# Query tiles' numerators one slot later, and first in TensorE's slot: a linear attention stage ahead of two expert layers

## The reference

```python
def phi(x):
    proj = np.einsum('bhsd,df->bhsf', x, w_phi)              # 64 -> 128 features
    proj = proj - np.max(np.abs(proj), axis=-1, keepdims=True)
    return np.concatenate([np.exp(proj), np.exp(-proj)], axis=-1)
q_p, k_p = (phi(q), phi(k))
kv = np.einsum('bhsf,bhsd->bhfd', k_p, v)
z = np.sum(k_p, axis=2)
num = np.einsum('bhsf,bhfd->bhsd', q_p, kv)
den = np.einsum('bhsf,bhf->bhs', q_p, z)[..., None] + 1e-06
return (num / den).astype(np.float32)
```

## Time and profile before

| | us |
|---|---|
| median of three runs | 910.85 (910.55 to 911.68) |
| the profiled execution, its own time | 910.34 |
| its span in the trace | 908.7 |
| TensorE busy, share of the span | 886.8, 98% |
| VectorE busy | 432.3, 48% |
| ScalarE busy | 293.9, 32% |
| GpSimd busy | 123.4, 14% |

### The profile page before, as it was taken

The page is one execution under the profiler, slowest core; times in us unless marked ns, Lnnn a source line. Parts: engine busy times, 40 slices in busy tenths (PEclk is TensorE's granted clock), DMA queues, the critical chain, the costliest instruction groups (busy, mean ns, idle before and its releaser), DMA issues.

```text
span 908.7 us, 15622 instructions
## 1 busy us (share of the span) xinstructions
PE 886.8 (98%) x5888; PEld 811.7 (89%) x5889; DVE 432.3 (48%) x875; ACT 293.9 (32%) x479; POOL 123.4 (14%) x145
## 2 busy tenths in 40 slices
PE   8999999999999999999999999999999999999996
PEld 6795968779999999999988999999999999999996
DVE  5678687898767644333457422222222222222222
ACT  4545454572155532223353321121112112112111
POOL 1010302122344112222300010010001001001001
PEclk9999999999999999999999999999999999999999
DMA  9513713112457432346743630030020002000000
GB/s 296 178 54 124 271 52 104 53 48 59 157 177 196 79 58 71 26 78 122 159 157 114 181 112 1 1 105 1 0 70 35 0 2 102 0 0 35 1 1 35
DMA packets 37181, 75.31 MB, mean 83 GB/s; under 512 B 8176, under 2 KB 24688, under 8 KB 35472
## 3 DMA queue, kind: packets, MB, share of 16 engines
q1 hardware_dynamic: 32832, 56.07, 23.2%
q0 software_dynamic: 3488, 17.85, 5.3%
q10 hardware_dynamic: 816, 0.79, 0.3%
HBM read 51.06 MB, written 23.64 MB: 82 GB/s over the span
## 4 chain that ended last, share of the span: by engine, by line
PE 89%; DVE 5%; issue 2%; ACT 2%; DMA 1%; POOL 0%; POOLq 0%; DVEq 0%; SPq 0%; ACTq 0%
PE ps L1023 10%; PE ps L1025 10%; PE ps L1024 10%; PE ps L822 6%; PE ps L1038 5%; PE ps L1039 5%; PE ps L1037 5%; PE ps L925 4%; PE ps L938 3%; PE ps L926 3%; PE ps L927 3%; PE ps L940 3%; PE ps L939 3%; PE ps L769 3%; PE ps L729 2%
## 5 line engine op out<-in xcount | busy, mean ns | idle before, releaser
L1023 PE MATMUL ps<-xnH,blkH 128*128 128x384 f32 x576 | 193.7, 336 | 3.0 <-DVE blkL L1690 1.9
L1025 PE MATMUL ps<-xnH,blkL 128*128 128x384 f32 x576 | 193.4, 336 | 0.0
L1024 PE MATMUL ps<-xnL,blkH 128*128 128x384 f32 x576 | 193.2, 335 | 0.0
L1697 DVE TENSOR_TENSOR sg<-sg,ps 128x384 f32<-128x384 f32 x72 | 39.8, 553 | 245.5 <-ACT sg L1256 241.6
L1256 ACT ACTIVATE sg<-ps 128x384 f32<-128x384 f32 x72 | 35.4, 491 | 252.1 <-PE ps L1025 252.1
L1023 PEld LDWEIGHTS ps<-xnH,blkH 128*128 128x128 f32 x576 | 108.2, 188 | 7.5 <-issue 4.3
L1024 PEld LDWEIGHTS ps<-xnL,blkH 128*128 128x128 f32 x576 | 108.2, 188 | 2.6
L1025 PEld LDWEIGHTS ps<-xnH,blkL 128*128 128x128 f32 x576 | 108.1, 188 | 0.0
L1038 PE MATMUL ps<-blkL,hH 128*128 128x512 f32 x216 | 84.8, 393 | 0.0
L1039 PE MATMUL ps<-blkH,hL 128*128 128x512 f32 x216 | 84.8, 392 | 0.0
L1037 PE MATMUL ps<-blkH,hH 128*128 128x512 f32 x216 | 84.5, 391 | 0.0
(11 more groups left out here) (219 smaller groups left out, 1593.6 us busy)
## 6 DMA issues: line engine op xcount, KB each, us to landing
stage<-in_ffn_w SPq DMA_DIRECT2D x12, 768.0 KB, 4.3
xin<-xs_dram SPq DMA_DIRECT2D x9, 578.2 KB, 9.9
xs_dram<-zrow SPq DMA_DIRECT2D x8, 578.2 KB, 8.6
qT<-in_q SPq DMA_DIRECT2D x4, 1152.0 KB, 5.5
xnH_dram<-xoH SPq DMA_DIRECT2D x8, 576.0 KB, 3.5
xnL_dram<-xoL SPq DMA_DIRECT2D x8, 576.0 KB, 6.1
xnH<-xnH_dram SPq DMA_DIRECT2D x6, 768.0 KB, 5.4
xnL<-xnL_dram SPq DMA_DIRECT2D x6, 768.0 KB, 6.3
```

Source lines behind the costliest of these rows:

```text
L1023: e.matmul(o, hi, xnH[par][:, c, :], start=(c == 0), stop=False)
L1024: e.matmul(o, hi, xnL[par][:, c, :], start=False, stop=False)
L1025: last = e.matmul(o, lo, xnH[par][:, c, :], start=False, stop=(c == KC - 1))
```

## The change

- `num_of`: the packed tile's numerators go to bank 2, one of the transposes' banks, and no longer to bank 6.
- TensorE: the numerators of a tile come three slots after its own (`g3`) and not two, as first half, projections, second half, ahead of the key sums and transposes. The packed tile's numerators (slot 2 of the next batch) stand between the two halves' projections with nothing between their own halves, and the second half's projections come ahead of the key sums there. In all other slots the second half's projections come last. Slot 7 has no numerators any more.
- VectorE: normalises the tile of four slots ago.
- The second wait in `key_sums` is gone; the first transposes of a batch wait for the previous batch's last normalisation in its place.
- The splits of the last batch move from its slots 1, 2, 5, 6, 7, 8, 9 to 2, 4, 5, 7, 8, 8, 9.
- The hand-over: `first_transposes` uses its banks in another order, waits for one tile of exponentials less, and for the last tile only ahead of bank 2. The numerators of slot 8's tile now come behind the first transposes, in `slot(B, 1)`, and the packed tile's behind the wait for `dve_XT`, in `slot(B, 2)`.

```diff
@@ num_of
-            first = KVB if at[1] % NJ % 2 == 1 else ZB
+            first = 2 if packed(at) else KVB if at[1] % NJ % 2 == 1 else ZB
@@
-        split_slots_dve = [(B - 1, sl) for sl in (1, 2, 5, 6, 7, 8, 9)] + [(B, 0)]
+        split_slots_dve = [(B - 1, sl) for sl in (2, 4, 5, 7, 8, 8, 9)] + [(B, 0)]
-        XT_FIRST = (2, 3, 1, 0)
+        XT_FIRST = (3, 1, 0, 2)
@@ key_sums
-                if j == 0 and not first:
-                    e.wait_ge(s["dve_N"], at[0] * NJ)
-                    settle(e, "carry_pe")
@@ numerators
-                    elif at[1] > NJ + 1:
+                    elif at[1] > NJ + 1 and not packed(at):
@@ TensorE's slot
-                g1, g2 = (before_slot(b, sl, n) for n in (1, 2))
+                g1, g2, g3 = (before_slot(b, sl, n) for n in (1, 2, 3))
-                turned = sl == NJ + 2 and has_slot(b)
-                if turned:
+                short = is_q(g3) and packed(g3)
+                if sl == NJ + 2 and has_slot(b):
                     turn(b)
+                if is_q(g3) and not short:
+                    numerators(g3, 0)
                 if has_slot(b):
                     projections(b, sl, 0)
+                if short:
+                    numerators(g3, 0)
+                if is_q(g3):
+                    numerators(g3, 1)
+                if short and has_slot(b):
+                    projections(b, sl, 1)
                 if is_k(g2):
                     key_sums(g2)
...
                     elif not (isinstance(g1[0], int) and g1[0] == 0):
                         e.wait_ge(s["act_Q"], g1[0] * NJ)
+                        e.wait_ge(s["dve_N"], g1[0] * NJ)
+                        settle(e, "carry_pe")
...
-                if is_q(g2) and not turned:
-                    numerators(g2, 0)
-                if has_slot(b):
+                if has_slot(b) and not short:
                     projections(b, sl, 1)
-                if turned:
-                    numerators(g2, 0)
-                if is_q(g2):
-                    numerators(g2, 1)
@@ first_transposes
                 for c in range(KC):
+                    if c == KC - 1:
+                        e.wait_ge(s["act_Q"], B * NJ)
                     x_transpose(c, XT_FIRST[c])
@@ hand-over, TensorE
-                e.wait_ge(s["act_Q"], B * NJ)
+                e.wait_ge(s["act_Q"], B * NJ - 1)
                 first_transposes()
             slot(B, 1)
             with e.If(early > 0):
                 e.wait_ge(s["dve_XT"], KC)
+            slot(B, 2)
+            with e.If(early > 0):
                 once(0, 0)
                 hidden(0, 0, 0)
...
-            for sl in range(2, TAIL_SLOTS):
+            for sl in range(3, TAIL_SLOTS):
@@ VectorE's slot
-                g3 = before_slot(b, sl, 3)
+                g4 = before_slot(b, sl, 4)
                 if sl == NJ + 2 and has_slot(b):
                     turned_evac(b)
-                if is_q(g3):
-                    normalise(g3)
+                if is_q(g4):
+                    normalise(g4)
...
-                    n = split_slots_dve.index((b, sl))
-                    split_low(n, 0, n + 1)
+                    for n, at in enumerate(split_slots_dve):
+                        if at == (b, sl):
+                            split_low(n, 0, n + 1)
```

## The result

| | before | after |
|---|---|---|
| median of 8 runs each, same chips | 910.58 us | 914.56 us |
| lowest to highest | 909.9 to 911.68 | 913.13 to 916.32 |
| ratio, 95% interval | | 1.0043 [1.0033, 1.0054] |
| profiled execution, time (span) | 910.34 (908.7) | 915.47 (913.9) |
| mean granted clock of TensorE, profiled | 0.999 | 0.988 |

The forecast was 908.9 us, the range 906.4 to 911.2. What came is rival (c), to which the prediction gave 0.06: 913.8 forecast for it, 914.56 measured.

The account below looks back on a forecast made before the run. TensorE, busy 98% at full clock, was taken as the bound. Gains of 4.7 + 1.2 us, less 0.9 + 0.6 at and after the borders and 2.5 at the hand-over, made 1.9 us less: 908.9 us, range 906.4 to 911.2.

Parts of the forecast that it names:

- rival (c): Idle time ahead of the first transposes drops TensorE's clock to 1.2 GHz; numerators behind take twice as long, 913.8 us; chance 0.06.
- The borders: At three borders between batches, TensorE's waits lose 4.6 to 4.7 us; the change leaves 0.9 us of that.
- the second waits: TensorE's slot 3 waits for a low part at the borders, 0.29 us at the one shown; they would go.
- The new order on TensorE: Fewer entries into fast runs and packed numerators in one run save 0.4 us a border, 1.2 us in all.
- The last batch: Moved splits delay VectorE: slot 5's projections 0.25 us late, `turn` 0.35 us late, 0.6 us more in all.
- The hand-over's wait: Ahead of the experts' first transposes TensorE idles 3.1 us, from 217.08 us until they start at 220.2 us.
- my chain of 12.65 us: VectorE's steps without pause from 203.42 us until slot 6's rows are normalised at 216.1 us.
- Nothing overlaps: At the hand-over, GpSimd's copy (0.6), VectorE's last split (1.14) and the gating (2.03) run one after another, until 220.0 us.
- the term of the hand-over: At the hand-over to the experts, `hidden` starts 1.85 us later, plus a 0.65 us wait: 2.5 us lost.
- The 0.65 us for `early_low(0)`: After two chunks of hidden rows, TensorE waits 0.65 us for VectorE's late `early_low(0)`.
- (a): The hand-over hides: transposes start near 218.5 us, loss there under 1 us, time 907.1 us; chance 0.22.
- (b): Waits move and don't go: half the border gain, 2.2 us, comes back as waits, time 911.1 us; chance 0.22.

Follow-up runs that it names:

- experiment 1: The changed kernel with 29 extra fast matmuls, results unused, ahead of the first transposes; 908.03 us against 909.31 for the kernel before.
- experiment 4: The changed kernel with the numerators of slot 8's tile back ahead of the first transposes; 905.65 us against 909.31 for the kernel before.
- experiment 3: The changed kernel with the last batch's splits back in slots 1, 2, 5, 6, 7, 8, 9; 910.9 us, 1.0008 of the kernel before.
- experiment 6: The kernel of experiment 4 with the packed numerators back in bank 6 and the key sums' second wait restored; 916.45 us, 1.0084 of the kernel before.
- experiment 2: The changed kernel with GpSimd gating the experts' first rows ahead of copying slot 6's tile; 910.94 us, 1.0013 of the kernel before.
- experiment 5: The kernel before, with GpSimd's gating put behind the copies of three tiles and not two; 911.78 us against 909.35.
- experiment 7: The changed kernel with 15 extra fast matmuls, results unused, ahead of the first transposes; 912.51 us, 1.0035 of the kernel before.
- experiment 9: The changed kernel with 16 extra fast matmuls, results unused, right behind the first transposes; 912.96 us, 1.0035 of the kernel before.

## Why the prediction was wrong, point by point

**The borders: right.** "Left over at the borders: 3 x 0.3 = 0.9 us" measured 0.19, 0.22 and none, 0.41 in all; the second waits and that for a normalised tile went. Counted between the key sums of each border (15.79, 72.64, 125.38 and 179.26 us before; 17.07, 72.55, 124.05 and 175.54 after) the three gained 1.37, 1.24 and 2.39 us, 5.0 in all, and the forecast had 4.7 + 1.2 - 0.9 = 5.0. **The new order on TensorE: nearly right.** Of these 5.0 us, 3.6 are the waits that the rows show (3.99 before, 0.41 after). By the prediction's figures for what the idle column misses, 0.66 us before and 0.32 after, 1.1 us is left for the order (an estimate), for 1.2. **The last batch: somewhat more than forecast.** "0.6 us more" measured 0.77. In slot 5 the projections came 0.50 us later behind the key sums than before (the 0.43 shown, and a little that the idle column misses), where 0.25 was forecast. And `turn` was late as well, though no wait is printed for it:

```profile
192.91 0.28 PE L731 MATMUL ps<-wbdH,tL 128*128 128x256 f32 x1
193.31 1.32 PE L787 MATMUL ps<-kvI,kvT 128*128 128x160 f32 x8
```

It starts 0.40 us after the product before it and not 0.12, so 0.28 us late for a forecast of 0.35; VectorE's copy of the sums ends at 193.16. The whole stretch gained 4.23 us for a forecast of 4.7 + 1.2 - 0.9 - 0.6 = 4.4: this part of the sum was right, term by term.

**The hand-over's wait: nearly right.** From slot 6's tile to the start of the transposes I had 4.1 us (216.1 to 220.2); it was 3.89 (213.99 to 217.88). GpSimd's timeline:

```profile
214.15 0.61 POOL L596 COPY x5s<-x 128x512 f32<-128x512 f32 x1 [3.45 <-DVE x L1367]
215.22 2.52 POOL L621 TENSOR_SCALAR xin<-xin 96x512 f32<-96x512 f32 x3 [0.46 <-issue]
```

Copy, then gating, as forecast. "Nothing overlaps" was too strict: the split beside them took 1.66 us in place of 1.22, and the gating 2.52 in place of 2.03, but the gating (from 215.22) started before the split had ended (215.84). TensorE waited 3.59 us and not 3.1, chiefly because VectorE came later than my chain of 12.65 us "with no pause": 13.49 us, with one pause in it.

```profile
200.50 0.68 DVE L1313 TENSOR_REDUCE mx<-ps 128x4 f32<-128x512 f32 x1
...
202.68 0.69 DVE L1313 TENSOR_REDUCE mx<-ps 128x4 f32<-128x512 f32 x1 [0.77 <-PE ps L731]
...
213.31 0.68 DVE L1367 TENSOR_TENSOR x<-ps,rd 128x512 f32<-128x512 f32 x1
...
214.18 1.66 DVE L1455 TENSOR_TENSOR w2L<-w2raw,w2H 128x1024 fp32r<-128x1024 f32 x1
```

The profile puts the 0.77 us down to TensorE's projections, but those had ended by 201.4. What held VectorE is open; in experiments 1 and 4, which don't have the pause, slot 6's tile is normalised some 0.9 us earlier against TensorE's work.

**The failed step: "Then transposes 1.09, numerators of slot 8's tile 3.53, packed numerators 1.37", the term of the hand-over in the sum.** It put a gap of 3.1 us ahead of them and left their full-speed lengths standing. They took 1.95, 6.94 and 2.36. Without the half speed the hand-over up to `hidden` would have lost 7.75 - 5.26 = 2.5 us, for 1.85 forecast. So the wait was mis-sized by 0.6, and the work behind it by 5.3.

**The rival was right and its chance wrong.** Rival (c) named place and mechanism, and its price of 4.9 us, doubling the two runs of numerators, measured 4.4 for those, with 0.9 for the transposes and 0.5 for `hidden` on top. Its chance of 0.06 rested on the clock being full "also with 1.29 us idle". But that gap has the dense products of `hidden` right behind it, and the 1.67 us of experiment 4 has them close behind, whereas mine was more than twice as long, with transposes and numerators behind. A row for a short gap in one surrounding is not evidence on a long one in another. The Trainium skill, page "TensorE: Matmul & The Clock Gate", section "Part 1: The HAM clock gate", has idleness bring the clock down and steady work bring it up; the trace after agrees with the first by the fall at 216.6. On the second it shows 12.4 us of work without a pause before the rise, 6.94 of them numerators.

**The rest.** The 0.65 us for `early_low(0)` did not show in the changed kernel, where no such wait is printed, perhaps because the slow numerators gave VectorE time; it did show where the clock held: 0.66 in experiment 1, 0.7 in experiment 3. Rivals (a) and (b) did not happen. With the clock held the change alone gives 908.03, against the kernel before's 909.31 on that chip, so -1.3 us where the forecast was -1.9: the mechanism of the forecast stood, and its sum was right to 0.6 us apart from the clock (experiment 1 holds the clock with filling, so this is the nearest measurement of it and not the thing itself). Experiment 4, which beats both kernels, keeps all of the change but the place of one tile's numerators.

Open: what decides whether the clock falls (experiment 6 shows both outcomes for one length of gap; experiments 2, 3 and 5 show both for one kernel, with the gap of the low ones not traced), what brings it back, why VectorE paused, and why the start of the kernel fell to half speed in one profiled execution.

## What to carry to other kernels

Before work is moved away from a place where one stage hands over to the next, ask what TensorE has in its queue there: a gap of 3.6 us, in place of a later one of 1.3 us, lost 2.5 us as waiting and 5.3 us again in the work behind it, which is more than the 4.2 us that the change had won in the rest of its stage. Where such a gap has no dense products right behind it, price the clock in the main sum and not in a rival, and fill the gap by moving a block of work that exists already: here the place of 32 matmuls is worth 7.6 us (4.0 above the kernel before in the changed kernel, 3.7 below it in experiment 4). And when a kernel's runs fall into two groups, read the mean granted clock of each run beside its time.

## What the runs showed of the hardware

- The clock fell with a gap of 3.6 us ahead of float32 transposes and numerators in every run of the changed kernel (8 of 8), and with one of 1.78 us in 5 of 5 (experiment 7), both by the mean clock of each run. The kernel of experiment 2 had 1.98 us and a full clock in its profile; in 9 of its 12 runs the mean clock was low, with a gap that was not traced. With 1.67 us and `hidden`'s products close behind, the mean stayed at 0.996 to 0.998 in all 5 runs (experiment 4), as in the kernel before. One gap of 2.08 us was followed by a fall and another was not, in one execution (experiment 6).
- The fall came inside the gap (216.6, changed kernel), during the transposes behind it (217.0, experiment 7) or with the first fast products (218.0, experiment 9): a full clock at the end of a gap does not mean that it has been survived.
- It stayed low for 13.7, 10.2 and 3.4 us in these three, and for 3.4 us twice in experiment 6.
- VectorE's split and GpSimd's work are longer when they meet: the split took 1.66 us (changed kernel) and 1.82 us (kernel before) for 1.22 alone, and the gating 2.52 to 3.11 us for 2.03. In the kernel before, where the split began 1.29 us into the gating, the gating kept its 2.03 us and the copy behind it took 1.59 for about 0.6.
